# Early places and late low halves for the first weights, both heads' states in one instruction, and the first unit's gates on VectorE, in a kernel of gated attention and two feed-forward layers

## The reference

```
f = 1 / (1 + exp(-f_logit))                                # gated linear attention, per head
state = f[t] * state + outer(k[t], v[t]); y[t] = q[t] @ state      # 32 heads, 768 steps, 48 x 48
x = y as (3072, 384)
x = ((x @ w_a) * (x @ w_b)) @ w_out                        # first layer, 384 -> 1536 -> 384
p = domain_probs / (sum(domain_probs) + 1e-9)
out = sum over e of p[:, e] * (max(x @ w1[e], 0) @ w2[e])  # second layer, 4 x (384 -> 1024 -> 384)
```

## Time and profile before

| | before |
|---|---|
| median of 3 runs | 1343.7 us (1343.36 to 1343.78) |
| the profiled execution, its own time | 1343.41 us |
| span of the profiled execution | 1341.7 us |
| PE busy | 1325.3 us, 99% |
| DVE, ACT, POOL busy | 863.7, 602.0, 574.1 us |
| mean granted clock of PE | 0.997 |

### The profile page before, as it was taken

The page is one execution under the profiler, slowest core; times in us unless marked ns, Lnnn a source line. Parts: engine busy times, 40 slices in busy tenths (PEclk is TensorE's granted clock), DMA queues, the critical chain, the costliest instruction groups (busy, mean ns, idle before and its releaser), DMA issues.

```text
span 1341.7 us, 23409 instructions
## 1 busy us (share of the span) xinstructions
PE 1325.3 (99%) x8187; PEld 1298.7 (97%) x8187; DVE 863.7 (64%) x1681; ACT 602.0 (45%) x1227; POOL 574.1 (43%) x575
## 2 busy tenths in 40 slices
PE   8899999999999999999999999999999999999998
PEld 7799999999999999999999999999999999999998
DVE  8776556656543333346777687777777776777765
ACT  4544434434332222344445654545554446454541
POOL 4442212313115767224444644445644447544441
PEclk9999999999999999999999999999999999999999
DMA  6543223222202434212222333332243322342221
GB/s 166 158 113 65 67 45 67 62 50 67 54 10 93 126 111 125 89 57 95 84 88 77 89 100 125 96 95 77 89 130 95 94 75 73 115 126 89 88 65 48
DMA packets 80166, 118.77 MB, mean 89 GB/s; under 512 B 8112, under 2 KB 61872, under 8 KB 80048
## 3 DMA queue, kind: packets, MB, share of 16 engines
q1 hardware_dynamic: 80048, 117.26, 30.6%
HBM read 100.58 MB, written 14.55 MB: 86 GB/s over the span
## 4 chain that ended last, share of the span: by engine, by line
PE 94%; DVE 1%; issue 1%; DMA 1%; ACT 1%; ACTq 0%; DVEq 0%; SPq 0%
PE bank L1677 12%; PE bank L1679 11%; PE bank L1678 11%; PE bank L1878 10%; PE bank L1879 10%; PE bank L1880 10%; PE bank L1772 8%; PE bank L1774 7%; PE bank L1773 7%; PE bank L1642 2%; PE bank L1672 2%; PE bank L1651 1%; PE bank L1665 1%; PE bank L1850 1%; PE bank L1849 1%
## 5 line engine op out<-in xcount | busy, mean ns | idle before, releaser
L1148 POOL TENSOR_TENSOR wu<-w_r,wu 128x640 fp32r<-128x640 f32 (+1 forms) x132 | 200.7, 1524 | 323.0 <-ACT wu L881 323.0
L1878 PE MATMUL bank<-wd,h_hi 128*128 128x384 f32 x768 | 259.7, 338 | 0.0
L1879 PE MATMUL bank<-wd,h_hi 128*128 128x384 f32 x768 | 257.7, 335 | 0.0
L1880 PE MATMUL bank<-wd,h_lo 128*128 128x384 f32 x768 | 257.2, 335 | 0.0
L1500 DVE SCALAR_TENSOR_TENSOR xt<-bank,pn,xt 128x384 f32<-128x384 f32 x288 | 177.0, 615 | 97.3 <-PE bank L1880 88.4
L908 ACT ACTIVATE h_hi<-h 128x384 fp32r<-128x384 f32 x240 | 124.7, 524 | 196.5 <-DVE h L1450 80.0
L1772 PE MATMUL bank<-x_hi,wu 128*128 128x384 f32 x600 | 202.0, 337 | 2.4 <-ACT h L896 1.4
L1774 PE MATMUL bank<-x_lo,wu 128*128 128x384 f32 x600 | 202.7, 338 | 0.0
L1773 PE MATMUL bank<-x_hi,wu 128*128 128x384 f32 x600 | 200.9, 335 | 0.0
L1677 PE MATMUL bank<-xs_hi,wab 128*128 128x384 f32 x576 | 196.1, 340 | 1.5 <-ACT xs_hi L867 1.3
L1678 PE MATMUL bank<-xs_hi,wab 128*128 128x384 f32 x576 | 193.2, 336 | 0.0
(11 more groups left out here) (137 smaller groups left out, 2494.0 us busy)
## 6 DMA issues: line engine op xcount, KB each, us to landing
w_r<-weight_sums SPq DMA_DIRECT2D x120, 320.0 KB, 2.9
raw<-w SPq DMA_DIRECT2D x48, 576.0 KB, 4.0
unit<-fkq SPq DMA_DIRECT2D x62, 216.0 KB, 4.2
v_in<-v_chunks SPq DMA_DIRECT2D x32, 144.0 KB, 3.9
out<-xt SPq DMA_DIRECT2D x24, 192.0 KB, 4.4
weight_sums<-w_s SPq DMA_DIRECT2D x10, 384.0 KB, 4.4
xt<-ystage SPq DMA_DIRECT2D x48, 72.0 KB, 2.2
weight_sums<-w SPq DMA_DIRECT2D x40, 64.0 KB, 2.7
```

Of the source, the lines that this page charges most:

```text
L1148: eng.tensor_tensor(wu_piece(g, n, 1), wu_raw(g, n), wu_piece(g, n, 0).bitcast(f32), ALU.subtract).then_inc(s_ulo, 1)
L1878: eng.matmul(o, hh, w_hi, start=(f == fs[0]), stop=False)
L1879: eng.matmul(o, hh, w_lo, start=False, stop=False)
L1880: mm = eng.matmul(o, hl, w_hi, start=False, stop=(f == fs[-1]))
```

## The change

Five things are altered.

- The first six pieces get places of their own, `raw_x` (in the tokens' second buffer) and `raw_w` (at the start of `wo_lo`), and semaphores of their own, so that their loads wait for nothing. Pieces 6 and 7 are loaded together at step `J[2] + 6`. Unit 5's load moves forward, to `J[0] + 6`.
- The high halves of pieces 0 to 5 are made at steps `J[0] + 4` to `+ 11`, and the low halves in the order 0, 1, 3, 4, 2, 5 at steps `LOW_AT`.
- `state` makes both heads' blocks with one instruction of 112 x 96, in an array whose columns 0 to 95 are used; `output` takes the state for each head apart, in a quarter of PE's array each.
- Unit 0's `gates` are made on DVE. For units 1 to 3 POOL makes the queries before the keys.
- Units 4 to 31 come 3 steps later; the idle products are 2 ahead of `turn`, 3 ahead of `kv`, 8 ahead of the layer and 6 inside `first_up_1`, behind a new wait for unit 3's copied result, where there were 5 ahead of `turn` and 15 ahead of the layer.

```diff
-    WARM_UP, AT_TURN, AT_FFN = 35, 5, 15
+    WARM_UP, AT_TURN, AT_KV, AT_FFN, AT_X = 35, 2, 3, 8, 6
...
-    J = [APART * (u - FIRST - 1) for u in range(FIRST)] + [PACE * (u - FIRST) + 2 for u in range(FIRST, NU)]
+    J = [APART * (u - FIRST - 1) for u in range(FIRST)] + [PACE * (u - FIRST) + 5 for u in range(FIRST, NU)]
...
-    NEXT = dict(APART_FROM, limit=-7, logs=-6, sums=-5, decays=-4, gates=-4, ends=-3, keys=-2)
+    NEXT = dict(APART_FROM, load=-20, limit=-7, logs=-6, sums=-5, decays=-4, gates=-4, ends=-2, keys=-2)
...
-            return J[0] + 1 + 9 * r // 5
-        return 2 * (r - R0)
+            return J[0] + (4, 5, 7, 8, 10, 11, 14)[r]
+        return 2 * (r - R0) + (3 if PIECES_1[r][0] == 2 and PIECES_1[r][2] * OPR >= FT1 // 2 else 0)
...
+    LOW_ORDER = (0, 1, 3, 4, 2, 5)
+    EARLY = len(LOW_ORDER)
+    LOW_AT = (J[0] + 8, J[0] + 11, J[0] + 13, J[0] + 11, J[0] + 11, J[0] + 14) + tuple(split_at(r) for r in range(EARLY, R1))
...
-        return (-3, -1, -1)[k] if n == 0 else 36 * (n - 1) + (29 if n == 1 else 20) + 2 * k
+        return k - 3 if n == 0 else 31 + k if n == 1 else 36 * (n - 1) + 20 + 2 * k
...
+        early = ExitStack()
+        sb(early, "to_xs_hi11", [128, attn_bytes // 4 + 2 * KT * TB1])
+        raw_x = sb(early, "raw_x", [128, EARLY // 2, PIECE])
+        sb(early, "to_wo_lo", [128, 4 * KT * F1 + FT1 * DM])
+        raw_w = sb(early, "raw_w", [128, EARLY // 2, PIECE])
...
+            else:
+                eng.wait_ge(s_wlo, EARLY)
...
             def load_raw(r):
-                if r >= 2:
+                if r >= EARLY + 2:
                     eng.wait_ge(s_whi, r - 1)
                     eng.wait_ge(s_wlo, r - 1)
...
-                eng.tensor_tensor(k, k, unit_ring[n][0:P2, F, :], ALU.mult).then_inc(s_kg, 1)
-                eng.wait_ge(s_dec, u + 1)
-                q = unit_ring[n][0:P2, Q, :]
-                eng.tensor_tensor(q, q, dec[0:P2, :], ALU.mult).then_inc(s_qg, 1)
+                if u < FIRST:
+                    eng.wait_ge(s_dec, u + 1)
+                    eng.tensor_tensor(q, q, dec[0:P2, :], ALU.mult).then_inc(s_qg, 1)
+                    eng.wait_ge(s_inv, u + 1)
+                    eng.tensor_tensor(k, k, unit_ring[n][0:P2, F, :], ALU.mult).then_inc(s_kg, 1)
...
+            def first_key_gate():
+                k = unit_ring[0][0:P2, K, :]
+                eng.wait_ge(s_inv, 1)
+                eng.wait_ge(s_in[0], 32)
+                eng.tensor_tensor(k, k, unit_ring[0][0:P2, F, :], ALU.mult).then_inc(s_kg, 1)
+
+            def first_query_gate():
+                q = unit_ring[0][0:P2, Q, :]
+                eng.tensor_tensor(q, q, dec[0:P2, :], ALU.mult).then_inc(s_qg, 1)
...
-                    for start, d0 in ((0, 0), (64, D)):
-                        new = st_after(u, cc)[start:start + D, start:start + D]
-                        old = st_before(u, cc)[start:start + D, start:start + D]
...
+                    new = st_after(u, cc)[0:P2, 0:2 * D]
+                    old = st_before(u, cc)[0:P2, 0:2 * D]
+                    kv = SETS[two(u)][0][0:P2, cc * 2 * D:(cc + 1) * 2 * D]
...
-                    eng.matmul(o[0:P2, t], st_before(u, cc)[0:P2, :], unit_ring[ring(u)][0:P2, Q, t],
-                               start=(cc == with_state[0]), stop=False, skip_group_check=True)
+                    for n, start in enumerate((0, 64)):
+                        eng.matmul(o[start:start + D, t], st_before(u, cc)[start:start + D, n * D:(n + 1) * D],
+                                   unit_ring[ring(u)][start:start + D, Q, t], start=(cc == with_state[0]), stop=False,
+                                   tile_position=(start, start), skip_group_check=True)
...
             def first_up_1():
                 for ks in (range(KT - 1), range(KT - 1, KT)):
+                    if ks[0]:
+                        eng.wait_ge(s_ys, FIRST)
+                        idle(SETS[1][0], AT_X)
```

More of the change, by code:

```diff
@@ L288, in gated_attention_then_two_ffns @@
         s_v = [sem(f"s_v{n}") for n in range(VRING)]
+        s_early = [sem(f"s_early{n}") for n in range(EARLY)]
         s_raw = [sem(f"s_raw{n}") for n in range(2)]
@@ L599, in states @@
                 done += CPU if half_of(x) < UPP - 1 else CPU - 1
-            return 2 * (done + n)
+            return done + n
         def is_strong(eng):
@@ L722, in _ @@
                     store_x(u)
-                if (u := at(j, "load")) is not None and u > FIRST:
+                if j == J[0] + 6:
+                    load_unit(FIRST + 1)
+                if (u := at(j, "load")) is not None and u > FIRST + 1:
                     load_unit(u)
@@ L726, in _ @@
                     load_v(u)
-                if j - 1 in SPLIT_AT and SPLIT_AT[j - 1] + 2 < R1:
+                if j == J[2] + 6:
+                    load_raw(EARLY)
+                    load_raw(EARLY + 1)
+                if j - 1 in SPLIT_AT and EARLY + 2 <= SPLIT_AT[j - 1] + 2 < R1:
                     load_raw(SPLIT_AT[j - 1] + 2)
@@ L1163, in _ @@
                     eng.memset(st_in[:, :, :, :], 0.0).then_inc(s_const, 1)
-                if (u := at(j, "gates")) is not None:
+                if (u := at(j, "gates")) is not None and u:
                     gates(u)
@@ L1389, in _ @@
                         eng.wait_ge(s_set, 6)
-                if j in SPLIT_AT and SPLIT_AT[j] < R0:
-                    first_lo(SPLIT_AT[j])
+                for r in sorted(range(R0), key=(LOW_ORDER + (EARLY,)).index):
+                    if j == LOW_AT[r]:
+                        first_lo(r)
                 for n in range(NXS):
@@ L1723, in down_1, with idle @@
                 mm.then_inc(s_down, 1)
-            def idle(count):
+            def idle(to, count):
                 for n in range(count):
-                    eng.matmul(bank[3][:, 0:128], ident[:, :], ident[:, :], start=True, stop=True)
+                    eng.matmul(to[:, 0:128], ident[:, :], ident[:, :], start=True, stop=True)
             eng.wait_ge(s_const, 2)
-            idle(WARM_UP)
+            idle(bank[3], WARM_UP)
             eng.wait_ge(s_set, 6)
@@ L1739, in _ @@
                     if i == 0 and part == 0:
-                        idle(AT_FFN)
+                        idle(bank[3], AT_FFN)
                         first_up_1()
@@ L1747, in _ @@
                     if 0 < u < FIRST:
-                        idle(AT_TURN)
+                        idle(bank[3], AT_TURN)
                     turn(u)
@@ L1754, in _ @@
                 if (u := at(j, "kv")) is not None:
+                    if u < FIRST:
+                        idle(bank[3], AT_KV)
                     kv(u)
```

53 lines of the change are left out of this document (35 added, 18 removed).

## The result

| | before | after |
|---|---|---|
| median of 5 runs, us | 1343.36 (1343.28 to 1343.78) | 1349.52 (1348.37 to 1349.90) |
| profiled execution: its time, its span | 1343.4, 1341.7 | 1349.5, 1347.7 |

A forecast was written before the change was run, and what follows sets the result against it. PE was taken to bound the kernel (busy 99% of the span), so time could be won only in its waits before some 54 us. 1343.4 - 3.8 (start) + 2.8 (state products) = 1342.4 us; range 1338.0 to 1346.8.

The forecast's parts named there:

- That is 2.3 us before the 32.51: Start, unit 2's output: ends at 30.2 us instead of 32.51, with unit 3's output following at once.
- 6.9 us are won here: Start, the layer's first slice: its last matmuls done at 40.6 us instead of 47.5.
- Part is given back: Between first slice and down_1(0): late gates and low half beside POOL; down_1(0) at 49.05, 4.55 us sooner than before.
- PE's clock falls to 1.2 GHz: Start, a gap near 43 us: part of the slow-start rival (0.14), 1.7 us of work if PE is full.
- the 3.8 us predicted: Net gain at the start after what is given back: 3.8 us, between 1.5 and 6.1.
- the start gives everything back: Slower rival, start: late gate(0), low halves or clock leave a lead of 0 to 1 us; 1346 to 1348, chance 0.14.
- 0.10 us for each unit, 2.8 us in 28 units: State products where PE is full: one more change of PE's shape, 0.13 less 0.03 for shorter passes; bounds 0 to 5.6.
- the serial quarters (1358): Slower rival, state products: both heads' matmuls take turns in one bank, 15.7 us more, 1358; chance 0.05.
- At no cost: Later stretch: DVE's 80 fewer instructions, units 3 steps later and 2 more idle products change nothing.
- For gates that are again late by the scans: Start: 0.3 us taken off the lead for gates late by unit 5's scans.
- `limit(3)`'s half chance: Start, DVE: limit(3) may get in between POOL's two operations; half this chance makes 6.9 us won 7.3.
- The bounds: Own range 1340.8 to 1345.5 (lead 1.5 to 5, price 2 to 4); whole range 1338.0 to 1346.8.

The follow-up runs named there:

- e4_later_splits: The changed kernel with pieces 8 to 14 split one to three steps later: 1344.44 us, ratio 1.0008.
- e3: The kernel before with only the change's states (both heads in one instruction) and state products in quarters of PE: 1346.53 us, ratio 1.0025.
- e1: The changed kernel with the weight sums (SUMS_AT) 3 steps earlier, at their step of before: 1347.09 us, ratio 1.0028.
- e7: The kernel before with only the weight sums' date (SUMS_AT) 3 steps later: 1344.77 us, ratio 1.0009.
- e2: The changed kernel with states and their products as before (one instruction per head, one matmul of 112 rows): 1344.80 us, ratio 1.0010.
- e9: The changed kernel with 14 more idle products in PE's wait ahead of down_1(0): 1346.04 us, ratio 1.0020.
- e12: e8 with unit 0's gates on POOL again, as before the change: 1340.63 us, ratio 0.9978.
- e5_halves: The kernel before with a state matmul for each head, on column halves of PE, states as before: 1343.49 us, ratio 1.0001.
- e8: The changed kernel with weight sums 3 steps earlier, states and outputs as before, pieces 8 to 14 split later: 1339.91 us, ratio 0.9971.
- e6: The changed kernel with 28 more idle products ahead of down_1(0): 1349.06 us, ratio 1.0038.
- e10: e8 with the change's own states and outputs (one instruction for both heads, quarters of PE): 1343.09 us, ratio 0.9997.
- e11: e8 with piece 7 also split later, at step 3 instead of 0: 1339.42 us, ratio 0.9970.

## Why the prediction was wrong

- **"That is 2.3 us before the 32.51. `output(3)` follows at once and ends at 31.5", "6.9 us are won here"**: right; 31.44, and the first slice's last products from 40.57. Early places, low halves behind the states and early gates together do what the sum said; but for the gates no run tells their shares. (Unit 3's output ended at 37.92 before and not at 37.8, which changes nothing.)
- **"Part is given back ... its low half on DVE falls beside POOL's piece 8, as it did at 51.63 (1.87 us): 49.0"**: this step failed. I counted one meeting with one operation of POOL, as the earlier trace rows show it. But I took `h_rest(0)` alone and left out what stands ahead of it, `keys(4)`, and that POOL's gate and two low halves follow each other without a gap. The result is 51.60 in place of 49.05, and a stretch at half clock behind the wait, which the text held to be a rival ("PE's clock falls to 1.2 GHz") and not a consequence: 2.55 + 1.6 us. That, of the 3.8 us predicted, left -0.4. e4_later_splits, which takes the two low halves out of this meeting, gets them back. The rival "the start gives everything back" (0.14) named this part, an order that makes the first low half late and the clock, with a right mechanism.
- **"0.10 us for each unit, 2.8 us in 28 units"**: right in kind, short in size; 0.13 and 3.6. The 0.03 taken off for shorter passes is not there (e3). "They should take one's time" held, so the serial quarters (1358) did not come.
- **"At no cost: ... units 3 steps later, as nothing that waits for them comes within 3 steps"**: this step failed. I looked for who waits for the units, and not for what has its date from them. The weight sums, 2.2 us at 551, were in no rival; e1 and e7 show it from both sides. Their slack was 4.7 us and the delay 4.7, so their slower rounds, which vary from execution to execution, are paid in full.
- **"DVE's 80 fewer instructions"**: at no gain, as said (e2).
- **"For gates that are again late by the scans" (0.3), `limit(3)`'s half chance (0.4)**: no run tells these apart.
- **The bounds** do not follow from their own terms: a lead of 0 and a price of 5.6 make 1349.0 and not 1348, a lead of 1.5 and a price of 4 make 1345.9 and not 1345.5. So the upper end of the range, 1346.8, left out more of the slow starts than it seems to, and even 1349.0 lies under the 1349.5 measured.

With the two failed steps and the size put right the sum is 1343.4 + 0.4 + 3.6 + 2.2 = 1349.6 against 1349.5.

## What to carry to other kernels

When work is moved forward so that a queue is met sooner, lay the two queues that hold each other beside each other over the whole of the new stretch and count all of the other's operations that follow without a gap, not one. When anything gets a later date, search the schedule for all that is dated from it: work that is far away and paced by itself can have been a few steps from lateness. And before two products are packed into another part of the array, count the changes of shape in the sequence, since each costs PE time that nothing hides where PE is full. Last, a gain read from one profile is to be split by place before it is given to one cause: in e9 and e12 differences of 0.6 us that look like the edit's had come from the landing of the tokens.

## What the runs showed of the hardware

- A waiting operation of DVE was passed over by POOL again and again: the keys, two operands in SBUF, 0.56 us alone, took 4.87 us beside three operations of POOL in a row (a gate of 1.00 and two low halves of 3.57 together), 4.88 in e9_warm_less, and 1.35 beside one in e4. After the change and in e4 alike it ends 0.42 us after the last of these operations (51.03 after 50.61, 47.04 after 46.62). The Trainium skill (SBUF — State Buffer, Who interferes with whom) says that a DVE instruction with two SBUF inputs contends with GpSimd instructions that read SBUF, and that the order of issue decides who blocks; the first agrees with these rows, and they add that POOL's next instruction comes before a DVE that waits already.
- Changing the shape of PE's division costs 0.13 us, from whole to halves (0.44 + 0.79 before, or 0.57 + 0.66 in e5_halves), from whole to quarters and from quarters to halves (0.57 + 0.79 in e3_quarters).
- PE's stretches at 1.2 GHz, 3.4 us each and in e1_sums once 6.8, began during or after waits within the first 60 us, and at places that differ from kernel to kernel: 41.3 and 51.6 after, 50.3 in e1_sums, 40.3 in e8, none after the warm-up in the profiles of e4, e6, e9, e10, e11 and e12. Where PE was full behind it, from `down_1(0)` to `(1)`, such a stretch cost 1.6 us (7.15 against 5.58 to 5.60 in e4, e6 and e9).
- These stretches do not explain how far the executions of one kernel lie apart, 2.1 to 4.3 us for e4, e8 and e11 and at most 1.3 for the kernel before. Nine of e4's eleven have a mean granted clock of 1.000, and these go from 1342.16 to 1345.34; all but one of e9's do, from 1345.11 to 1347.06. In e8's six alone the time goes with the clock (1338.3 and 1338.5 at 1.000, 1339.6 to 1340.3 at 0.999, 1340.8 at 0.997). Two other things differ between profiles whose program is the same up to there: the way from unit 3's copied result to its high half on ACT (3.7 us after, 3.5 in e6, 3.2 in e1 and e9) and the rounds of sums. How much of the spread is theirs no run shows.
